# One half step for two attention units, the 1e-9 by a pairwise sum, and two first loads issued by ScalarE, in a fused attention and expert kernel

## What is computed

```
scores = where(mask, q @ k.T / 8, -1e9)
attn = exp(scores - max(scores))
attn = attn / (sum(attn) + 1e-09)
x = attn @ v                               # heads side by side: 2304 x 512
h = x @ w_in                               # 512 -> 2048
g = h if h >= 1, 0 if h <= -1, else (h + 1)**2 / 4
x = g @ w_out
out = x; where x @ w_skip > 0: out = x + gate * (relu(x @ w1[e]) @ w2[e])
```

## Time and profile before

| | |
|---|---|
| median of the runs | 508.34 us (508.17 to 508.83) |
| the profiled execution | 509.94 us, span 508.1 us |
| PE busy | 497.4 us, 98% of the span |
| DVE busy | 260.7 us, 51% |
| POOL busy | 213.2 us, 42% |
| ACT busy | 195.5 us, 38% |
| chain that ended last | PE 85%, DVE 9%, issue 2%, ACT 2% |

### The profile page before, as it was taken

One profiled execution on the slowest core, in us unless ns is written; L12 is line 12 of the kernel. 1 busy time (PEld: TensorE's weight loads), 2 busy tenths in 40 slices (PEclk: granted clock), 3 DMA queues, 4 the chain that ended last, 5 costly groups with the idle time before them and its releaser, 6 DMA issues.

```text
span 508.1 us, 8892 instructions
## 1 busy us (share of the span) xinstructions
PE 497.4 (98%) x3423; PEld 428.7 (84%) x3423; DVE 260.7 (51%) x594; ACT 195.5 (38%) x435; POOL 213.2 (42%) x235
## 2 busy tenths in 40 slices
PE   8899999899999999999999999999999999999996
PEld 5577888789998888888888888888998899888895
DVE  5967557744335525676643676762435242332322
ACT  4776564462223334434332434433322222322222
POOL 0669777662223235455523546551222322222221
PEclk9799999999999999999999999999999999999999
DMA  8993202101101204020310420000210008750001
GB/s 254 337 386 136 76 2 79 53 2 72 54 0 50 73 23 168 13 73 32 97 48 0 173 80 18 17 1 19 88 37 1 1 9 323 275 182 1 2 1 65
DMA packets 18977, 42.15 MB, mean 83 GB/s; under 512 B 2054, under 2 KB 3920, under 8 KB 18932
## 3 DMA queue, kind: packets, MB, share of 16 engines
q1 hardware_dynamic: 18836, 41.54, 23.8%
q0 software_dynamic: 96, 0.02, 0.0%
HBM read 32.94 MB, written 8.78 MB: 82 GB/s over the span
## 4 chain that ended last, share of the span: by engine, by line
PE 85%; DVE 9%; issue 2%; ACT 2%; POOL 0%; DVEq 0%; ACTq 0%
PE bank L1029 36%; PE bank L1045 36%; PE bank L868 4%; PE bank L831 3%; PE bank L848 3%; DVE row_sum L1190 1%; PE bank L812 1%; DVE row_max L1168 1%; DVE x_lo L1200 1%; ACT x_hi L1575 1%; DVE row_sum L1193 1%; PE bank L972 1%; PE bank L953 1%; DVE act_f L1411 1%; DVE bank L1173 1%
## 5 line engine op out<-in xcount | busy, mean ns | idle before, releaser
L1780 POOL TENSOR_TENSOR g_lo<-act_f,g_hi 128x384 fp32r<-128x384 f32 x96 | 97.4, 1014 | 196.9 <-ACT g_hi L1677 196.5
L1668 ACT ACTIVATE act_f<-act_f,half_col 128x384 f32<-128x384 f32 x96 | 59.3, 617 | 201.5 <-DVE act_f L1411 201.5
L1411 DVE TENSOR_SCALAR act_f<-bank 128x384 f32<-128x384 f32 x96 | 53.2, 554 | 143.2 <-PE bank L1029 135.0
L1029 PE MATMUL bank<-x_hi,win_hi 128*128 128x384 f32 x384 | 87.8, 348 | 0.6 <-DVE act_f L1414 0.6
L1045 PE MATMUL bank<-wout_hi,g_hi 128*128 128x512 f32 x285 | 85.1, 407 | 0.0
L1677 ACT CAST g_hi<-act_f 128x384 fp32r<-128x384 f32 x96 | 49.4, 514 | 91.5 <-DVE act_f L1414 91.3
L1029 PE MATMUL bank<-x_hi,win_lo 128*128 128x384 f32 x384 | 83.9, 337 | 0.0
L1029 PE MATMUL bank<-x_lo,win_hi 128*128 128x384 f32 x384 | 83.1, 334 | 0.0
L1045 PE MATMUL bank<-wout_lo,g_hi 128*128 128x512 f32 x285 | 81.0, 392 | 0.0
L1045 PE MATMUL bank<-wout_hi,g_lo 128*128 128x512 f32 x285 | 81.0, 392 | 0.0
L1029 PEld LDWEIGHTS bank<-x_hi,win_hi 128*128 128x128 f32 x384 | 66.6, 188 | 8.5 <-issue 1.5
(11 more groups left out here) (129 smaller groups left out, 431.1 us busy)
## 6 DMA issues: line engine op xcount, KB each, us to landing
w_early<-in_w_dram SPq DMA_DIRECT2D x4, 2048.0 KB, 8.8
qk<-in_qk_dram SPq DMA_DIRECT2D x12, 592.0 KB, 4.6
out_dram<-y_rows SPq DMA_DIRECT2D x18, 256.0 KB, 2.6
win_raw<-in_w_in_dram SPq DMA_DIRECT2D x16, 256.0 KB, 9.3
wout_raw<-in_w_out_dram SPq DMA_DIRECT2D x16, 256.0 KB, 9.8
y_dram<-y_rows SPq DMA_DIRECT2D x15, 256.0 KB, 3.0
v<-in_v_dram SPq DMA_DIRECT2D x6, 384.0 KB
v<-in_v_dram SPq DMA_DIRECT2D x6, 288.0 KB
```

The lines of the kernel that those rows point to most:

```text
L1029: mm = pe.matmul(h_ps[s % 2][:, 0:CH], w[:, f, P * k:P * (k + 1)], x[:, k, cols], start=(at == 0), stop=(at == len(order) - 1))
L1411: dve.tensor_scalar(tile, h_ps[s % 2][:, 0:CH], -1.0, 1.0, ALU.max, ALU.min).then_inc(clip_ready, 1)
L1668: act.activation(tile, tile, ACT.Square, bias=half_col[:, 0:1], scale=0.5).then_inc(square_ready, 1)
L1780: pool.tensor_tensor(g_lo[:, s % RING, :], act_f[:, s % 2, :], g_hi[:, s % RING, :].bitcast(F32), ALU.subtract).then_inc(g_lo_ready, 1)
```

## The change

It has three parts.

- `FILLERS` gets four matmuls of ones ahead of the turning of unit 1. Unit 8 moves as a whole from half step 6 to 7. Unit 12's scores, exponentials and sums move from 21, 22 and 23 to 20, 21 and 22, while its P and V stay at 26 and 28.
- `reciprocal_sums` writes each row sum next to a 1e-9 that was set once at the start, and one TENSOR_REDUCE over the pairs takes the place of the TENSOR_SCALAR.
- ACT issues the load of the first pair's keys and that of the local mask, ahead of all its work, in place of SP.

```diff
-FILLERS = {("P", 0): 4, ("S", 1): 4, ("S", 2): 9, ("P", 2): 5, ...}
+FILLERS = {("P", 0): 4, ("S", 1): 4, ("S", 2): 9, ("P", 1): 4, ("P", 2): 5, ...}
...
-        for i, at in enumerate((6, 10, 14, 17, 21, 24)):
-            unit_at(N_PRO + REST + i, at, 5, 7)
+        for i, at in enumerate((7, 10, 14, 17, 20, 24)):
+            unit_at(N_PRO + REST + i, at, 6 if i == 4 else 5, 8 if i == 4 else 7)
...
+        sum_terms = sb("sum_terms", [TQ, 2, 4, 2], F32)
...
-            first_tiles(0)
-            constant(mask_l, "mask_local", mask_l_loaded)
+            sp.dma_start(qk_main[0][:, 0:4 * TQ], qk[0, 0, :, 0:4 * TQ]).then_inc(qk_loaded[0], 16)
             constant(ident, "ident", ident_loaded)
...
-                    dve.tensor_reduce(sums_of(u, hh), tiled(u, hh), AX.X, ALU.add).then_inc(sum_steps, 1)
+                    dve.tensor_reduce(sum_terms[0:unit_rows(u), hh, 0:u.nt, 0], tiled(u, hh), AX.X, ALU.add)\
+                       .then_inc(sum_steps, 1)
...
-                dve.tensor_scalar(sums, sums, 1e-9, None, ALU.add).then_inc(sum_steps, 1)
+                dve.tensor_reduce(sums, sum_terms[0:unit_rows(u), :, 0:u.nt, :], AX.X, ALU.add).then_inc(sum_steps, 1)
...
+            dve.memset(sum_terms[:, :, :, :], 1e-9).then_inc(terms_ready, 1)
+            dve.wait_ge(terms_ready, 1)
...
+            act.dma_start(qk_main[0][:, QC:QC + PAD + 4 * TQ], qk[0, 0, :, QC:QC + PAD + 4 * TQ])\
+               .then_inc(qk_loaded[0], 16)
+            at, rows, width = columns["mask_local"]
+            act.dma_start(mask_l[:, :], table_dram[0:rows, at:at + width]).then_inc(mask_l_loaded, 16)
```

More of the change, by code:

```diff
@@ L113 @@
 POOL_BEFORE = "G0 G1 G2 G3 G4 G5 R0 R1 R2"
-FILLERS = {("P", 0): 4, ("S", 1): 4, ("S", 2): 9, ("P", 2): 5, ("P", 3): 2, ("P", 4): 2, ("P", 5): 2, ("V", 4): 2}
+FILLERS = {("P", 0): 4, ("S", 1): 4, ("S", 2): 9, ("P", 1): 4, ("P", 2): 5, ("P", 3): 2, ("P", 4): 2, ("P", 5): 2, ("V", 4): 2}
 def jobs_of(names):
@@ L437, in build @@
         mask_l_loaded, mask_s_loaded = sem("mask_l_loaded"), sem("mask_s_loaded")
-        half_ready = sem("half_ready")
+        half_ready, terms_ready = sem("half_ready"), sem("terms_ready")
         warm_ready = sem("warm_ready")
```

## The result

The changed kernel takes 510.13 us (median of 10 runs, 509.63 to 510.47), the kernel before 508.54 (10 runs, 507.95 to 509.88): ratio 1.0027, 95% interval 1.0019 to 1.0035. The forecast was 506.1, faster. It is 1.6 us slower instead, and outside the range of 505.2 to 507.7.

The account below looks back on a forecast made before the run. PE, busy 98% of the span, was taken as the bound, its slow clock setting the prologue's end. Fillers -1.6, loads -0.1, 1e-9 +0.1 and half steps -0.6 gave -2.2: from the median 508.34 to 506.1 us, range 505.2 to 507.7.

Parts of the forecast that it names:

- Fillers: Prologue: four matmuls of ones fill PE's idle hole before unit 1's turning, the clock stays up, -1.6 us.
- Rival 1: Prologue: the clock falls all the same despite the added matmuls, 507.7 us; chance 12%.
- First loads: Start of the prologue: ACT issues the keys some 0.45 us earlier than SP did, worth only -0.1 us.
- rival 4: Start: the first loads land later, sharing the engines from two queues, up to +0.6, 506.7 us; chance 6%.
- The 1e-9: Row sums: TENSOR_REDUCE over 16 values takes as long as the short TENSOR_SCALARs plus a few hundredths, +0.1 us for all.
- Half steps: First chunk: moving units 8 and 12 removes two waits (-2.7) and adds three (+2.1), -0.6 us.
- three added waits: First chunk, PE: 0.5 us at unit 7's turning, 1.2 at unit 9's turning, 0.4 at unit 12's scores.
- both removed ones: First chunk, PE's waits: 1.0 us at unit 8's scores for keys, 1.7 at unit 11's turning for a bank.
- both terms: First chunk: the 1e-9 step's +0.1 us and the half steps' -0.6 us.
- rival 3: First chunk: the half steps give nothing, added waits being as large as removed ones, 506.7 to 507.2 us; chance 10%.
- Rival 2: Near 24 us: the clock falls later, into full PE work, losing 3.2 us, so 509.3 us; chance 5%.

Follow-up runs that it names:

- e6: Kernel before with one semaphore increment more on VectorE in step 70 and nothing else: 511.16 us, ratio 1.0043.
- e5: Changed kernel with the added 1e-9 memset issued by GpSimd instead of VectorE, whose program is again as long as before: 507.62 us, ratio 0.9982 to the kernel before.
- e7: Changed kernel with sixteen semaphore increments more on VectorE, one in each of steps 60 to 75: 507.95 us, ratio 0.9978 to the kernel before.
- e14: Kernel before with the four fillers and nothing else: 508.16 us, ratio 0.9985.
- e8: Kernel before with three semaphore increments more on TensorE, in steps 40 to 42: 508.36 us, ratio 0.9996.
- e15: Kernel before with the sum over pairs alone, its 1e-9 memset on GpSimd: 507.87 us, ratio 0.9980.

## Why the prediction was wrong

- **The end of the program.** "Behind the first chunk PE has no wait that the change touches, so the gain should stay whole to the end." This is the step that failed most, with 2.6 us. Up to left_i it held (-2.39 at hidden(16), -2.67 at left_i). What I didn't look at is the stretch behind left_i: 2.6 us in which nothing is busy, and of which the only record is four packets on the instruction queues. I costed the added memset as work on idle VectorE and not as one instruction more in its program (e6: one more on the kernel before, +2.7 us; e5: one fewer in the changed kernel, -2.5; e7: sixteen more, -2.2). No rival named it.
- **The sum against the median.** "It lies 1.6 above the median of the runs; from that, 508.34 - 2.2 = 506.1." The second failing step, with 1.5 us. The 1.6 by which the profiled execution was longer was the same 1.6 that the fillers were to give back: it had a slow stretch that two of three runs don't have. So the term was counted against a median that doesn't hold it. Measured on their own the fillers give 0.5 in the median. The right sum was 509.94 - 2.2 = 507.7 for the runs of that group, and for the rest, without the fillers' term, 508.4 - 0.6 = 507.8. e5, the change without its tail, measured 507.62. The tail adds 2.5 (510.13 less 507.62), and 506.1 + 1.5 + 2.5 is the 510.1 that was measured.
- **Fillers, -1.6 in the profiled execution.** hidden(0) came 1.79 earlier, -1.7 forecast with the loads, by the chain that I had followed (unit 2's copy at 21.56; I said 21.55). The size was right for a run with the long fall, which costs 1.6. That hidden(0) came out so close is in part luck, for among the kernels with fillers and ScalarE's loads it lies anywhere from 28.97 to 30.91. That the clock "then stays up" was wrong in this trace, since it fell 1.8 us earlier and for 3.4 us; in e14 it was right. Rival 1 had from the Trainium skill, "TensorE: Matmul & The Clock Gate", section "What's actually happening", that the activity is watched on a free-running count and the point of a change differs from run to run. That it differs the traces show: the clock fell at 17.0 in the kernel before and in e6 and not at all in e8, with the same code up to there; whether such a count is behind it, none shows. I had the consequence for the after and missed it for the before.
- **First loads, -0.1.** Wrong in sign by all three medians, +0.3: rival 4, at half its size. The first scores' weights were loaded at 4.50 and not at 4.11.
- **The 1e-9, +0.1.** Wrong: -1.1 (-0.8 in the chunk, -0.3 behind it). "What the long ones cost at 82.49 is hidden once unit 12's masking is ordered otherwise" was read in the new order only. In the old order the long step was 0.56 us of the very wait of 1.52 that I credited to the half steps (e15).
- **Half steps, -0.6.** The three added waits were right (0.43, 1.23, 0.54 for 0.5, 1.2, 0.4), both removed ones are gone, and the chunk is 0.60 shorter, where both terms together gave -0.5. Yet the credit was wrong: alone they are worth -0.5, beside the sum over pairs +0.2 (rival 3, that they give nothing, is the case). And the removed wait at unit 8 was read wrongly. "It is unit 8, whose keys come by a load that unit 6's scores release": those keys had landed 1.6 us before the wait began, and the wait was for ACT's copy of unit 6. Its size, 1.0, was right all the same. Two terms that take away the same wait were summed as if each had its own.
- **Rival 2** named the other side (509.3) by a later fall of the clock into full work, which no run showed.

Still open: why the clock falls in some runs of one program and not in others, why the late page goes with 3.0 us in e6 and 2.6 in the changed kernel, and where the edges of the pages lie.

## What to carry to other kernels

Before costing a term, see which kind of run the profile caught: where its time lies off the median by the size of the stall that you want to remove, that stall isn't in the median. When a program ends in a jump, the number of instructions ahead of it can have a price: read the packets of the instruction queues behind the last computation, and try one instruction more and some fewer before judging a change of 1 or 2 us. And where two parts of a change aim at the same wait, measure each with and without the other.

## What the hardware showed unexpectedly

- One semaphore increment on an engine with 51% load cost 2.7 us of 508 (e6), and a page of 8 KB more was fetched behind the last computation. Without that page, too, it is 2.6 to 2.7 us from left_i to the end in every version, with four pages fetched.
- The same program has two groups of times 1.5 us apart (508.4 and 509.9). The profiles of the longer kind have the clock at half for 6.8 us from 17.0 on, one of the shorter kind (e8) nowhere. With more work for TensorE, four matmuls of ones, no run of the longer kind is left (0 of 12).
- A TENSOR_SCALAR over 8 values took 1.23 us beside a TENSOR_TENSOR of GpSimd and ended with it, a TENSOR_REDUCE over 16 values at the same place 0.17. None of the 32 reductions of L1194 took more than 168 ns. That GpSimd holds the one and not the other fits both; no run moved GpSimd's instruction to show it.
